# The operands of a gated scan and ELU feed-forward kernel are placed 32 bytes further on in on-chip memory

## The reference

```python
sig = 1 / (1 + exp(-f_logit)); f = lower_bound + (1 - lower_bound) * sig
h[t] = f[t] * h[t-1] + (1 - f[t]) * x[t]          # per batch and channel, y[t] = h[t]
u = y.reshape(B * S, D) @ w_in                    # 12160 x 256 by 256 x 2048
g = where(u > 0, u, exp(min(u, 0)) - 1)           # ELU
out = g @ w_out                                   # 12160 x 2048 by 2048 x 256
```

## Time and profile before

| | before |
|---|---|
| median of 3 runs | 962.04 us |
| the profiled execution | 961.75 us |
| its span, first to last instruction | 959.9 us |
| PE busy | 954.5 us, 99% of the span |
| ACT, DVE, POOL busy | 82%, 75%, 66% |

### The profile page before, as it was taken

How to read it: one execution, slowest core, us unless ns; L and a number is a source line. 1 busy time by engine, 2 the same in 40 slices (tenths; PEclk the granted TensorE clock), 3 DMA queues, 4 the chain that set the end, 5 groups by cost and what they waited for, 6 DMA issues and landing times.

```text
span 959.9 us, 15015 instructions
## 1 busy us (share of the span) xinstructions
PE 954.5 (99%) x4362; PEld 815.6 (85%) x4362; DVE 722.9 (75%) x916; ACT 790.1 (82%) x1424; POOL 628.8 (66%) x475
## 2 busy tenths in 40 slices
PE   9999999999999999999999999999999999999998
PEld 6999888888888888888888888888888888888887
DVE  6998976976886796697688679678768867966444
ACT  7989888878888888888888888888888788887775
POOL 2588796576667668557656755856775765676544
PEclk9999999999999999999999999999999999999999
DMA  7212012002102201100210210120021021001001
GB/s 273 68 33 95 1 33 66 34 1 78 55 1 57 76 1 44 55 33 2 74 55 0 66 66 0 46 66 18 23 65 44 0 76 55 0 0 46 1 1 45
DMA packets 23078, 42.02 MB, mean 44 GB/s; under 512 B 2560, under 2 KB 4096, under 8 KB 23040
## 3 DMA queue, kind: packets, MB, share of 16 engines
q1 hardware_dynamic: 22752, 41.10, 13.2%
q10 hardware_dynamic: 288, 0.46, 0.2%
HBM read 29.10 MB, written 12.45 MB: 43 GB/s over the span
## 4 chain that ended last, share of the span: by engine, by line
PE 95%; ACT 2%; DVE 1%; issue 0%; DMA 0%; ACTq 0%; DVEq 0%
PE acc L893 17%; PE acc L895 17%; PE acc L894 17%; PE h L863 14%; PE h L865 14%; PE h L864 14%; ACT e L469 1%; PE h L998 1%; PE h L1000 1%; PE h L999 1%; ACT e L463 1%; DMA opening<-first_gate 0%; DVE x L625 0%; ACT opening L419 0%; PE h L964 0%
## 5 line engine op out<-in xcount | busy, mean ns | idle before, releaser
L335 POOL TENSOR_TENSOR g_lo<-e,g_hi 128x512 fp32r<-128x512 f32 (+1 forms) x384 | 516.6, 1356 | 325.2 <-ACT g_hi L477 323.8
L463 ACT ACTIVATE e<-h 128x512 f32<-128x512 f32 (+1 forms) x379 | 224.9, 594 | 124.3 <-PE h L865 90.1
L716 DVE SCALAR_TENSOR_TENSOR e<-e,h 128x512 f32<-128x512 f32 (+1 forms) x379 | 256.8, 677 | 70.2 <-ACT e L469 69.0
L893 PE MATMUL acc<-g_hi,w_out_hi 128*128 128x512 f32 (+1 forms) x768 | 291.1, 379 | 0.4 <-DVE w_out_lo L687 0.4
L895 PE MATMUL acc<-g_hi,w_out_lo 128*128 128x512 f32 (+1 forms) x768 | 291.0, 379 | 0.0
L894 PE MATMUL acc<-g_lo,w_out_hi 128*128 128x512 f32 (+1 forms) x768 | 290.9, 379 | 0.0
L469 ACT ACTIVATE e<-e 128x512 f32<-128x512 f32 (+1 forms) x384 | 241.2, 628 | 9.6 <-issue 1.1
L477 ACT CAST g_hi<-e 128x512 fp32r<-128x512 f32 (+1 forms) x384 | 232.0, 604 | 19.4 <-DVE e L716 19.4
L863 PE MATMUL h<-a_hi,w_in_hi 128*128 128x512 f32 x616 | 234.7, 381 | 0.0
L865 PE MATMUL h<-a_hi,w_in_lo 128*128 128x512 f32 x616 | 234.7, 381 | 0.0
L864 PE MATMUL h<-a_lo,w_in_hi 128*128 128x512 f32 x616 | 234.7, 381 | 0.0
(11 more groups left out here) (75 smaller groups left out, 555.8 us busy)
## 6 DMA issues: line engine op xcount, KB each, us to landing
opening<-forget_logit SPq DMA_DIRECT2D x44, 256.0 KB, 2.6
x<-value SPq DMA_DIRECT2D x44, 256.0 KB, 2.7
out<-out_sb SPq DMA_DIRECT2D x44, 256.0 KB, 2.0
w_in_raw<-w_in SPq DMA_DIRECT2D x8, 256.0 KB, 5.5
w_out_raw<-w_out SPq DMA_DIRECT2D x8, 256.0 KB, 6.6
out<-out_sb SPq DMA_DIRECT2D x4, 224.0 KB, 2.1
x<-value SPq DMA_DIRECT2D x3, 224.0 KB, 6.3
opening<-forget_logit SPq DMA_DIRECT2D x2, 224.0 KB, 6.4
```

The costliest lines, as they stand in the source:

```text
L335: nc.gpsimd.tensor_tensor(g_lo[:, t % RING, 0:w], e[:, t % TILES, 0:w], g_hi[:, t % RING, 0:w].bitcast(F32), ALU.subtract).then_inc(g_lo_r ...
L463: nc.scalar.activation(e[:, i, 0:w], bank_of(j, t)[:, 0:w], ACT.Relu, scale=-1.0).then_inc(r_ready, 1)
L716: nc.vector.scalar_tensor_tensor(e[:, t % TILES, 0:w], e[:, t % TILES, 0:w], -1.0, bank_of(j, t)[:, 0:w], ALU.add, ALU.max).then_inc(g_rea ...
L893: nc.tensor.matmul(bank, hi, g_h, start=opens, stop=False)
```

## The change

An unused tensor of 8 float32 numbers, 32 bytes of a partition, is allocated behind `x` and ahead of `a_hi`:

```diff
         x = sb("x", [P, BATCH, HALVES, TILE])
+        sb("room_of_rows", [P, 8])
         a_hi_at = -(-nc.sbuf_base // 32) * 32
         a_hi = sb("a_hi", [P, 2, PRODUCTS - 1, TILE], F32R)
         a_lo_at = -(-nc.sbuf_base // 32) * 32
         a_lo = sb("a_lo", [P, 2, PRODUCTS - 1, TILE], F32R)
```

## The result

The changed kernel takes **1007.95 us** (median of 6 runs, 1007.54 to 1008.18) against 961.84 us of the kernel before in the same comparison (961.46 to 962.39). The ratio is 1.048, with a 95% interval of 1.047 to 1.049: slower by 4.8%. I had forecast 948.7 us, with a range that ended at 990.

The account below looks back on a forecast made before the run. The prediction took PE, busy throughout, as the bound: matmuls times their distance. 4056 matmuls x 3.3 ns = 13.4 us off the profiled 961.75 gave 948.4, and 948.7 us for the median; the range was 942 to 990.

Parts of the forecast that it names:

- the long stretch: From 66.54 us to the end: PE runs 4056 matmuls without idle time; the forecast expected that to stay so.
- The price of a nanosecond: From 66.54 us on, one nanosecond per matmul is worth 4056 x 1 ns = 4.06 us.
- the rival that the address doesn't matter: All matmuls: the excess over the columns' time is a fixed price; no change, 962.0 us; chance 0.28.
- From this I take it that part of the 6.7 ns is reads in each other's way: Matmuls from 66.54 us on: row and weight reads disturb each other, costing 3.3 ns each, 13.4 us in all.
- the 6.7 ns: Matmuls of 512 columns: start-to-start distance of 220.0 ns less the columns' own 213.3 ns at 2.4 GHz.
- the slow matmuls after a standstill: Matmuls from 66.55 us, mostly 200 to 220 ns where 193.6 is the rule; read as showing distance isn't fixed.
- the 3.3 ns: Forecast gain per matmul from 66.54 us on: fp32r's 220.0 less the bf16 row's 216.7 ns.
- The rival of the fixed price: All matmuls: 6.7 ns over for 512 columns, 6.9 for 448, look fixed; no change, 962.0 us; chance 0.28.
- The count of meetings: Row and weights share a line modulo 512 bytes four times per load before, never with rows two lines on.
- the present relation is the quiet one: Rival for all 4344 fp32r matmuls: 220.0 is free of collisions, the new place slower; 28 us, 990 us; chance 0.30.
- the lowest level after the standstill: After 66.55 us: 200 against 193.6 ns, 6.4 ns more; for 4344 matmuls 28 us, 990 us.
- The next level: After 66.55 us: 207 to 210 ns; would make 58 to 71 us more, 1020 to 1033 us.

Follow-up runs that it names:

- both32: Weights, rows and everything else 32 bytes on against the kernel before, so rows and weights are again at the same place modulo 512 bytes; 961.62 us, ratio 0.9998.
- the probe: In place of the kernel, only PE's stream in groups of 40 matmuls, without gates, scan, ELU and both products; 512 columns took 220.0 ns or more per matmul.
- g32: Only the rows of the second product (g_hi, g_lo) 32 bytes on, against the kernel before; 1000.5 us, ratio 1.041.
- lo32: Only the rests of the weights (w_in_lo, w_out_lo) 32 bytes on, against the kernel before; 1004.7 us, ratio 1.045.
- the three probes: PE's matmul stream alone, 96 groups each: the kernel's and left-to-right reading orders, other orders, and standstills of varied length; 512 columns took 220.0 ns or more per matmul.
- rows256: Only the rows 256 bytes (sixteen lines) on, against the kernel before; 961.2 to 965.2 us, ratio 1.0003.
- rows64: Only the rows 64 bytes (four lines) on, against the kernel before; 988.2 us in one execution.
- weights32: Only the weights 32 bytes on, against the kernel before, so the rows lie two lines before the weights; 989.2 us in one execution.
- rows128: Only the rows 128 bytes (eight lines) on, against the kernel before; 1000.9 us in one execution.

## Why the prediction was wrong

**What held.** The bound: time is matmuls times distance, PE stays without idle time in the long stretch, nobody else limits it, the stretch up to 66 us changes by under 2 us. The price of a nanosecond, 4.06 us: 11.0 ns make 44.7. The relation of rows and weights does decide, against the rival that the address doesn't matter. both32 leaves only how the moved tensors lie to the others, and the probe, in which no other engine works beside PE, leaves only the rows and the weights. The rule of the Trainium skill (SBUF — State Buffer, Who interferes with whom) that PE never waits on anyone would have made 962 us; measured are 1008. That the two streams of reads wait for each other in the memory fits, but is not shown: no run took the loads away.

**The step that failed** is the one that begins "From this I take it that part of the 6.7 ns is reads in each other's way". I had one row on each side, the bf16 matmuls at 216.7 and the slow matmuls after a standstill at 199 to 216 for 193.6, and took the first as what the fp32r stream would reach without meetings. In 288 groups of the three probes, eight orders of reading and 16 relations, 512 columns never settled below 220.0, nor 448 below about 193.3. So the 3.3 ns were not there: in everything that was tried the 6.7 ns are the least that fp32r has, and the kernel before had nothing to win by moving its rows. What the runs showed in place of the gain is the loss of the quiet state, 11.0 ns more per matmul. bf16 was the wrong neighbour. It differed in its type and bytes, in reading one row of zeros, and in the order; the order isn't what made it quick, since fp32r rows from left to right had 226.7 at least. Which of the others is, no run shows. The Trainium skill's 215.7 ns (TensorE: Matmul & The Clock Gate, Wait — 56ns, not 53.3ns?) agrees with the bf16 rows and was reached by no fp32r group.

The rival of the fixed price rested on the equal excess at 448 and 512 columns, 6.9 and 6.7 ns. That reading proves no floor either: the changed kernel has 18.2 and 17.8 ns, nearly equal as well.

**The count of meetings** carried the sign. It assumed a common start, a pace, a period of 512 bytes and independent matmuls. It expected relation 4 to be like 0, which is 26 us off; the period is 256 bytes; and g32 and lo32 show that matmuls aren't independent.

**The rival that won**, the present relation is the quiet one, was right that 220.0 is the undisturbed distance and that the new place leaves the stream at a slower one, and the little disturbed loads were the row that spoke for it. That each matmul meets the weights, its reason, is not shown. Its price was too low: I took the lowest level after the standstill, 6.4 ns, and cut the range there at 990. Measured are 11.0 ns. The next level, 207 to 210 ns, was in the same rows and would have set the edge at 1020 or more. Nearly all of the 11.0 ns is the loss of the quiet state: the other state of relation 0 has about 230.7 in the probe.

## What to carry to other kernels

When PE is busy throughout, divide a long stretch by its matmuls before anything else. How far the distance lies over the columns' own time can depend on where the rows lie to the weights. Neither an equal excess for different numbers of columns nor a perfectly even stream shows that it is at its floor: at relation 2 the probe runs evenly at 230.0, 10 ns above the 220.0 of relation 13. Only other relations, measured beside it, show that. A layout in which rows and weights keep one relation throughout is worth a probe with all 16 relations and several starts each, one program, before a kernel is moved; a relation that is quiet from nearly every start (13 lines here, 27 of 28 groups) is worth more than one that is quiet from some (0 lines, 10 of 28).

## What the runs showed that I had not expected

- One program at one set of addresses has two steady distances, 220.0 and about 231 ns, and can change from one to the other in the midst of a stream (rows256 at 882.90 us).
- The steady patterns of the kernels add up to whole multiples of 6.67 ns: 220.0 is 33, 193.3 is 29, the three of the changed kernel 104 together, those of rows64 and weights32 102, the seven of rows128 241. The even 230.0 of the probe at relation 2 is 34.5 of them, so it takes two matmuls to a whole number. At 2.4 GHz 512 columns by themselves are 32, and 448 are 28. What sets this step no run shows.
